# A gated mixture of experts behind an attention stage: table reads moved to the head of each tile, half a weight matrix asked for after the hidden rows' way back, four fill products less

## What is computed

```python
for b in range(B):                       # 4
    prev_e = -1
    for s in range(S):                   # 576
        fresh_e = int(np.argmax(logits[b, s]))
        if s == 0 or local_gate[b, s] < 0.5:
            e = fresh_e
        else:
            e = prev_e if prev_e >= 0 else fresh_e
        prev_e = e
        ...
        h = np.maximum(x[b, s] @ w1[e], 0.0)      # 512 -> 1024
        out[b, s] = p[e] * (h @ w2[e])            # 1024 -> 512
```

## Time and profile before

| | |
|---|---|
| median of 3 runs | 449.35 us (448.23 to 450.46) |
| profiled execution, its own time | 446.81 us |
| its span | 445.1 us |
| mean granted clock of TensorE | 0.99 |
| TensorE (PE) busy | 423.7 us, 95% of the span |
| VectorE (DVE) busy | 304.0 us, 68% |
| ScalarE (ACT) busy | 228.8 us, 51% |
| GpSimd (POOL) busy | 306.3 us, 69% |

### The profile page before, as it was taken

One profiled execution on the slowest core, in us unless ns is written; L12 is line 12 of the kernel. 1 busy time (PEld: TensorE's weight loads), 2 busy tenths in 40 slices (PEclk: granted clock), 3 DMA queues, 4 the chain that ended last, 5 costly groups with the idle time before them and its releaser, 6 DMA issues.

```text
span 445.1 us, 13699 instructions
## 1 busy us (share of the span) xinstructions
PE 423.7 (95%) x3938; PEld 338.3 (76%) x3939; DVE 304.0 (68%) x502; ACT 228.8 (51%) x399; POOL 306.3 (69%) x324
## 2 busy tenths in 40 slices
PE   7999999999989989999999999999988979999992
PEld 3888888888768735788888878888867868888882
DVE  5678887887866687875872783786386877847440
ACT  3778777777777313263542742453273656435210
POOL 6877777877889404788777577687678767776421
PEclk9999999999999998999999999999999999999997
DMA  8989999999695675457779759968959999784430
GB/s 173 195 172 196 176 195 172 188 183 194 108 300 139 143 267 186 128 147 238 250 219 343 224 174 306 294 192 268 319 190 278 332 309 325 230 250 139 155 98 34
DMA packets 105740, 93.78 MB, mean 211 GB/s; under 512 B 49430, under 2 KB 84246, under 8 KB 105688
## 3 DMA queue, kind: packets, MB, share of 16 engines
q1 hardware_dynamic: 99960, 81.91, 69.8%
q0 software_dynamic: 5728, 11.30, 8.4%
HBM read 71.66 MB, written 22.82 MB: 212 GB/s over the span
## 4 chain that ended last, share of the span: by engine, by line
PE 72%; DMA 10%; DVE 8%; issue 3%; ACT 3%; SPq 2%; DVEq 1%; ACTq 1%; POOL 0%; POOLq 0%
PE psum L1689 39%; DMA h_part<-h_rows 5%; PE psum L1413 5%; PE psum L1486 4%; PE psum L1395 4%; DMA h_rows<-tile_bufs 3%; PE psum L1501 3%; PE psum L1449 2%; PE psum L1515 2%; PE psum L1423 2%; PE psum L1579 2%; DVE w_ring L1272 2%; PE psum L1472 2%; PE psum L1462 2%; PE psum L1590 2%
## 5 line engine op out<-in xcount | busy, mean ns | idle before, releaser
L749 POOL DMA_INDIRECT tile_bufs<-x_rows,from_part x96 | 128.4, 1337 | 49.2 <-issue 26.5
L1689 PE MATMUL psum<-w_ring,xg_t 128*128 x552 | 130.4, 392 | 2.9 <-DVE w_ring L1272 2.3
L1689 PE MATMUL psum<-w_ring,h_t 128*128 x552 | 130.2, 392 | 2.8 <-DVE w_ring L1272 2.3
L1689 PEld LDWEIGHTS psum<-w_ring,xg_t 128*128 128x128 f32 x552 | 103.2, 188 | 26.9 <-issue 5.3
L1689 PEld LDWEIGHTS psum<-w_ring,h_t 128*128 128x128 f32 x552 | 103.5, 188 | 26.2 <-issue 3.8
L1272 DVE TENSOR_TENSOR w_ring<-w_ring (+1 forms) x28 | 63.4, 2292 | 28.7 <-ACT w_ring L927 21.9
L970 ACT CAST h_t<-h_raw 128x512 fp32r<-128x512 f32 x46 | 27.3, 621 | 65.9 <-DVE h_raw L1298 65.9
L1298 DVE STREAM_TRANSPOSE h_raw<-h_part 128x512 f32<-128x512 f32 x46 | 29.9, 688 | 41.7 <-DMA h_part<-h_rows 41.7
L755 POOL DMA_INDIRECT out<-tile_bufs,to_row x23 | 29.9, 1301 | 25.5 <-DVE tile_bufs L1313 18.4
L962 ACT ACTIVATE tile_bufs<-psum 128x512 f32<-128x512 f32 x46 | 24.9, 594 | 40.5 <-PE psum L1689 38.3
L927 ACT CAST w_ring<-w_ring (+1 forms) x14 | 26.6, 1910 | 17.8 <-issue 14.7
(11 more groups left out here) (186 smaller groups left out, 620.7 us busy)
## 6 DMA issues: line engine op xcount, KB each, us to landing
w_ring<-moe_w SPq DMA_DIRECT2D x28, 1024.0 KB, 8.9
h_rows<-tile_bufs SPq DMA_DIRECT2D x46, 256.0 KB
h_part<-h_rows SPq DMA_DIRECT2D x92, 128.0 KB
early<-q SPq DMA_DIRECT2D x32, 144.0 KB, 4.1
early<-k SPq DMA_DIRECT2D x32, 144.0 KB, 4.0
early<-v SPq DMA_DIRECT2D x16, 288.0 KB
x_rows<-early SPq DMA_DIRECT2D x48, 96.0 KB, 2.6
early<-v SPq DMA_DIRECT2D x32, 120.0 KB
```

Of the source, the lines that this page charges most:

```text
L749: pool.indirect_dma_start(xg[:, t % 2, s * 128:(s + 1) * 128], None, x_parts[:, :], bass.IndirectOffsetOnAxis(from_part[:, t, s:s + 1], 0) ...
L1689: ins = mm(bank[b][:, :], rows, w_ring[:, bass.ds(at + (off + c * width + n * 512), 512)], start=(c == 0 and k == 0), stop=(c == chunks - ...
```

## The change

Three edits. SP, ScalarE and VectorE read all table entries of a tile at its head, ahead of all its work, instead of one by one ahead of each part that they decide; the reads of the late half of W2, W1 and the early half are kept in registers until used. In SP's `tile` the issue of `rest` stands behind `h_back` and no longer behind `h_store`. `WARM_TILES` is 18 instead of 22. TensorE's program is otherwise the same.

```diff
-    WARM, WARM_FIRST, WARM_CODES, WARM_HELD, WARM_TILES = 8, 4, 10, 4, 22
+    WARM, WARM_FIRST, WARM_CODES, WARM_HELD, WARM_TILES = 8, 4, 10, 4, 18
...
             def tile(t, par, w1=True, w2=True, rest=None):
 
+                if w1:
+                    next_w1 = next_of(t + 1)
+                if w2:
+                    next_w2 = next_of(t - 1)
                 h_store(t, par)
-                if rest:
-                    load_half_w2(1, par, *rest)
...
                 if w1:
 
-                    e, at = next_of(t + 1)
-                    load_next(load_w1, s_w1_in, 1 - par, e, at, 0, 1)
+                    load_next(load_w1, s_w1_in, 1 - par, *next_w1, 0, 1)
                 h_back(t, par)
+                if rest:
+                    load_half_w2(1, par, *rest)
                 if w1:
-                    load_next(load_w1, s_w1_in, 1 - par, e, at, 1, PIECES)
+                    load_next(load_w1, s_w1_in, 1 - par, *next_w1, 1, PIECES)
                 if w2:
 
-                    e, at = next_of(t - 1)
                     wait(sp, s_y, t - 1)
-                    load_half_w2(0, 1 - par, e, at)
-                    return e, at
+                    load_half_w2(0, 1 - par, *next_w2)
+                    return next_w2
...
-            def half_next_w2(t, piece, par, tiles):
+            def next_of(t):
 
-                e = act.value_load(tab_next[0:1, one(t)], min_val=0, max_val=E - 1)
+                return (act.value_load(tab_next[0:1, one(t)], min_val=0, max_val=E - 1),
+                        act.value_load(tab_next_w[0:1, one(t)], min_val=0, max_val=PLACE))
+
+            def half_next_w2(whose, piece, par, tiles):
+
+                e, at = whose
                 with act.If(e != 0):
-                    half_w2_hi(piece, par, tiles, act.value_load(tab_next_w[0:1, one(t)], min_val=0, max_val=PLACE))
+                    half_w2_hi(piece, par, tiles, at)
...
             def tile(t, par, half, x=True, w=True, late=True):
 
+                if late:
+                    late_w2 = next_of(t - 3)
+                if w:
+                    next_w1 = next_of(t)
+                next_w2 = next_of(t - 2)
                 relu(t, par)
                 h_hi(t - 1, 1 - par)
                 if x:
                     x_hi(t + 2, par)
 
                 if late:
-                    half_next_w2(t - 3, 1, 1 - par, half - 1 + par)
+                    half_next_w2(late_w2, 1, 1 - par, half - 1 + par)
                 if w:
-                    split_next_hi(t, half + 1, s_w1_in[par], s_w1_hi, 0, W1C)
-                half_next_w2(t - 2, 0, par, half)
+                    split_next_hi(next_w1, half + 1, s_w1_in[par], s_w1_hi, 0, W1C)
+                half_next_w2(next_w2, 0, par, half)
```

More of the change, by code:

```diff
@@ L928, in half_w2_hi, with split_next_hi @@
                                w_ring[:, bass.ds(at + (WCOLS + W1C + piece * n), n)].bitcast(F32)).then_inc(s_w2_hi, 1)
-            def half_next_w2(t, piece, par, tiles):
-                e = act.value_load(tab_next[0:1, one(t)], min_val=0, max_val=E - 1)
+            def next_of(t):
[3 more added lines that the diff above has]
+                e, at = whose
                 with act.If(e != 0):
-                    half_w2_hi(piece, par, tiles, act.value_load(tab_next_w[0:1, one(t)], min_val=0, max_val=PLACE))
-            def split_next_hi(t, tiles, s_in, s_hi, at, cols):
-                e = act.value_load(tab_next[0:1, one(t)], min_val=0, max_val=E - 1)
+                    half_w2_hi(piece, par, tiles, at)
+            def split_next_hi(whose, tiles, s_in, s_hi, at, cols):
+                e, place = whose
                 with act.If(e != 0):
-                    split_hi(s_in, s_hi, tiles,
-                             act.value_load(tab_next_w[0:1, one(t)], min_val=0, max_val=PLACE) + at, cols)
+                    split_hi(s_in, s_hi, tiles, place + at, cols)
             def first_x_hi():
@@ L988, in _ @@
             x_hi(3, 1)
-            split_next_hi(1, 1, s_w1_in[1], s_w1_hi, 0, W1C)
+            split_next_hi(next_of(1), 1, s_w1_in[1], s_w1_hi, 0, W1C)
             for i in range(PIECES):
@@ L1018, in _ @@
                     h_hi(t - 1, (t - 1) % 2)
-                    half_next_w2(t - 3, 1, (t - 1) % 2, (t - 1) // 2)
+                    half_next_w2(next_of(t - 3), 1, (t - 1) % 2, (t - 1) // 2)
                     for i in range(PIECES):
-                        half_next_w2(t - 2, i, t % 2, t // 2)
+                        half_next_w2(next_of(t - 2), i, t % 2, t // 2)
         @block.vector
@@ L1273, in split_lo, with next_of, split_next_lo @@
                                             ALU.subtract).then_inc(s_lo, 1)
-            def split_next_lo(t, s_hi, s_lo, at, cols, first=0, end=PIECES):
-                e = dve.value_load(tab_next[0:1, one(t)], min_val=0, max_val=E - 1)
+            def next_of(t):
+                return (dve.value_load(tab_next[0:1, one(t)], min_val=0, max_val=E - 1),
+                        dve.value_load(tab_next_w[0:1, one(t)], min_val=0, max_val=PLACE))
+            def split_next_lo(whose, s_hi, s_lo, at, cols, first=0, end=PIECES):
+                e, place = whose
                 with dve.If(e != 0):
-                    split_lo(s_hi, s_lo, e,
-                             dve.value_load(tab_next_w[0:1, one(t)], min_val=0, max_val=PLACE) + at, cols, first, end)
+                    split_lo(s_hi, s_lo, e, place + at, cols, first, end)
             def x_tr(t, par, came):
@@ L1326, in tile @@
                 if late:
-                    split_next_lo(t - 3, s_w2_hi, s_w2, W1C, W2C, 1, PIECES)
+                    split_next_lo(late_w2, s_w2_hi, s_w2, W1C, W2C, 1, PIECES)
                 y_scale(t - 2, par, half)
                 if w:
-                    split_next_lo(t, s_w1_hi, s_w1, 0, W1C)
-                split_next_lo(t - 2, s_w2_hi, s_w2, W1C, W2C, 0, 1)
+                    split_next_lo(next_w1, s_w1_hi, s_w1, 0, W1C)
+                split_next_lo(next_w2, s_w2_hi, s_w2, W1C, W2C, 0, 1)
             x_tr(1, 1, 1)
@@ L1365, in _ @@
             x_lo(3, 1)
-            split_next_lo(1, s_w1_hi, s_w1, 0, W1C)
+            split_next_lo(next_of(1), s_w1_hi, s_w1, 0, W1C)
             split_lo(s_w2_hi, s_w2, 1, PLACE + W1C, W2C)
@@ L1381, in _ @@
                     h_lo(t - 1, (t - 1) % 2)
-                    split_next_lo(t - 3, s_w2_hi, s_w2, W1C, W2C, 1, PIECES)
+                    split_next_lo(next_of(t - 3), s_w2_hi, s_w2, W1C, W2C, 1, PIECES)
                     y_scale(t - 2, t % 2, t // 2 - 1)
-                    split_next_lo(t - 2, s_w2_hi, s_w2, W1C, W2C)
+                    split_next_lo(next_of(t - 2), s_w2_hi, s_w2, W1C, W2C)
                     y_scale(t - 1, (t - 1) % 2, (t - 1) // 2)
```

## The result

Over 20 executions each, the changed kernel has a median of 453.75 us (448.47 to 457.43) and the kernel before 449.05 (447.32 to 458.05). The ratio is 1.0059, 95% interval 1.0031 to 1.0087: slower by 0.6%. The forecast was 443.3, with a range up to 447.4.

The account below looks back on a forecast made before the run. TensorE was busy 95% of the span, so only its idle time at three breaks could be won. -6.3 (breaks) + 0.4 (S(17)) - 0.1 (fills) = -6.0 us from the 449.35 median gave 443.3, range 440.3 to 447.4.

Parts of the forecast that it names:

- I book the reads at nothing by themselves, and 0.8 us more slack at every break.: Reads at tile heads were taken as covered by waits, costing nothing; SP's earlier W1 issue adds 0.8 us slack.
- F(2): First product of slot tile 2; four fills less were to bring it at most 0.24 us, booked as 0.1.
- S(17): Second product of slot tile 17, with 0.3 us of slack before the change; a loss of 0.4 was booked.
- ScalarE's row of 0.89: ScalarE's 0.89 us idle on issue between x cast and late-half weight cast, to vanish with the reads moved.
- The heads of the tiles are not covered: Rival, chance 0.06: six reads ahead of relu and the h_part transpose cost up to 3.3 us each; time 453.
- S(15): Second product of slot tile 15, the third break: 2.45 us lost before, waiting for the second matrix's split.
- F(15): First product of slot tile 15, the second break: 2.51 us lost before, to be covered by 3.2 won.
- SP's order at S(6): First break, second product of slot tile 6: rest behind h_part wins 3.2 us against 0.61 lost; the wait goes.
- Break three goes, or a remnant of up to 1 us stays: At S(15), h_part lands 3.5 us earlier and the rest near 357, so its 2.45 us loss goes or nearly.
- The late half of W2 becomes the bound: Rival, chance 0.17: rest 2 to 3 us later, S(15) keeps 2.45, S(17) waits 1; time 446.8.
- The fills: Four fill products fewer before the first products: worth 0.8 us there, of which 0.1 was booked.
- The sum: Over the whole kernel: -6.3 (breaks and after-effects) + 0.4 (S(17)) - 0.1 (fills) = -6.0 us.

Follow-up runs that it names:

- i1: VectorE's reads at the heads of the tiles and nothing else, against the kernel before: ratio 1.0303.
- i2: VectorE's and ScalarE's reads at the heads; SP, order and fills as in the kernel before: ratio 1.0087 to it.
- e2: The kernel before with only the rest issued behind h_back instead of behind h_store: ratio 0.9904 to the kernel before.
- f3: The order alone again, the same edit as e2, in another group: ratio 0.9931 to the kernel before.
- h3: The changed kernel with ScalarE's reads back where they stood: ratio 1.0188 to the kernel before.
- g2: The new order of SP and 18 fills, all reads where they stood before: ratio 0.9961 to the kernel before.
- h4: g2 again in another group, order and 18 fills with no read moved: ratio 0.9940 to the kernel before.
- g3: The changed kernel with the rest back behind the store, so reads at the heads and 18 fills: ratio 1.0033 to the kernel before.
- g1: The changed kernel with 22 fills instead of 18, so reads at the heads and the new order: ratio 0.9977 to the kernel before.
- f1_after: The changed kernel measured again: median 472.30 us, ratio 1.0060 to the kernel before.
- h1: The changed kernel measured again in another group: median 467.41 us, ratio 1.0014 to the kernel before.

## Why the prediction was wrong, step by step

- **"I book the reads at nothing by themselves, and 0.8 us more slack at every break."** This is the step that failed. A head was to cost up to 3.3 us only where it is not covered, with "up to 1 us of lateness" in tiles without weights. It is uncovered on VectorE in 14 tiles at 2.6 us and on ScalarE in 13 at 2.1, and every kernel of the table above with moved reads takes 3.8 us or more longer from F(2) to the end. The queue does run ahead, but not far enough. This is the chain after, ahead of S(17):

```profile
381.39 0.31 DVEq L1397
...
382.10 0.30 DVEq L1290
...
382.72 0.30 DVEq L1291
...
383.69 0.30 DVEq L1290
...
384.30 0.30 DVEq L1291
...
384.91 0.31 DVEq L1290
...
385.53 0.31 DVEq L1291
```

The three splits before it work until 384.29 (they began at 377.60 and take 6.69). L1397 is the read of the number of tiles in use, which stands once behind the loop in both kernels, at 381.39, 2.9 us under the splits. The six reads of the head (L1290 and L1291 in turn) start at 382.10, 2.2 us under them. A read mostly follows the last one by 0.61 us, and the six take 4.1; the transposition starts at 386.23, 1.9 after the splits' end. My single row of a read under a working engine showed that cover exists, not how much of it. The Trainium skill, "DMA: Bandwidth & Descriptors", section "Latency and other measured facts", has about 600 ns as the floor of a tensor_load. The pace here, 0.61 with the register work, comes out at that, though the load's own row is 0.30 to 0.31. My 0.55 was a little low.

- **What the reads left.** I looked at where the reads go and not at what covered them where they stood. VectorE's were free there, in the wait for ScalarE's cast. I had credited only ScalarE's row of 0.89. i1 against i2 shows both sides: VectorE's move costs 3.0%, ScalarE's gives 2.1% back.
- **The slower rival, "The heads of the tiles are not covered"**, had the right place, a price near the measured one (2 to 3 us at breaks; S(15) lost 3.3 more, S(17) 2.1, F(15) gained 0.5) and a time of 453, which is what came, at a chance of 0.06. That its time fits so well is in part luck: its 10 us were to fall on four places, and fell mostly on S(15), the product behind it and S(17). My evidence against it was again that one row.
- **SP's order at S(6): right.** h_part was transposed at 242.80 (before 245.48), the late half cast at 246.06 (2.9 sooner than in the earlier trace rows; the sum said 3.6), and the wait is gone, though not in e2, f3 and h3 (0.8 to 1.9 late). At F(15) it is right in g2 (0.5 lost) and e2 (0.1), and not in f3 and h4 (4.0 and 4.9 lost), for which I have no cause; in the changed kernel F(15) still loses 2.05.
- **"Break three goes, or a remnant of up to 1 us stays": wrong even for the order alone.** The rest was issued at 351.75 in g2, as worked out (351.8), but landed at 359.3 and not near 357: I gave it a slot of 3.4 to 4 behind h_part, and it took 7.5 us from issue to landing. (No row shows the 1.8 us that I gave h_part at the least; the shortest landing that the list of issues of the trace before gives is 2.0.) S(15) kept its loss (3.0), S(17) lost 1.6 and not 0.4. That is the first rival, "The late half of W2 becomes the bound", in the numbers it gave: break three kept, a wait of 1 at S(17). In the mechanism it is right at S(15) only; at S(17) in g2 it was the store issued behind the rest, which took 6.00 us, where my sum had a slot of 1.5, read from no row. The rival's -2.6 us is also near g2's measured -0.4% (1.8 us), but that is not borne out: by g2's own profile breaks and after-effects took 0.5 us more than before, not 2.6 less. Where its 0.4% comes from is not shown.
- **The two rivals met, in one profile.** Behind h_back the rest hangs on relu and the store. In the profile after, relu's reads made the store of that tile 2.5 us later than before, and the rest 2.3 later than in g2; it also landed 0.8 us more slowly, and S(15) loses 5.74 instead of 3.0. Without the new order (g3) the weights of S(15) are ready 3.9 us sooner after F(15). But g1, with the same reads and order, loses no more at S(15) than g2. That the meeting costs something beyond the two parts is argued from these traces, not shown. How the parts add up stays open too: the reads of all three engines alone gave 0.9971 and 0.9949 on chips with pauses, and with 18 fills on a chip without them 1.0033, while without SP's (i2) they gave 1.0087. SP's own heads or the chips may be the difference; no run had SP's heads alone, and none had all reads alone on a chip without pauses.
- **The fills: right that they are worth nothing** (1.0035, an interval that takes in 1, and the same 19.73 us from the first fill to F(2)). The 18 took 4.07 us, 0.23 each against 0.30 before, the granted clock from 176 to 189 was 1.00, and F(2) started at 188.5.
- **The sum** took each break from the execution profiled before and moved it. No term was for a chain that is free today becoming late, apart from the 0.4 at S(17), and that is where 3.3 (S(15)) + 1.7 (behind it) + 2.1 (S(17)) of the loss came from.

The version that beats both kernels is the order without the reads: 0.9904 and 0.9931 with 22 fills, 0.9961 and 0.9940 with 18. The last two are the firmer ones, as their medians of all executions say the same (0.4 and 0.8% below before).

## What to carry to other kernels

Before moving a small instruction to a "free" place, ask what covers it where it stands: VectorE's reads in the shadow of a wait cost nothing here, and the same reads ahead of the engine's first work of a tile stopped it for 2.6 us on average in 14 tiles. A transfer that is issued behind another step is issued late when that step is late, so an edit that delays relu and an edit that puts a load behind relu's store must be judged together. And time the parts of a change apart: here one of three was worth 0.4 to 1.0% by the ratios, and the reads hid it.

## What the runs showed of the hardware

Long waits of TensorE cost more than their length here. These are the windows of the changed kernel around S(15) (stretch: us, busy time and instructions of PE, PEld, DVE, ACT, POOL, granted clock, DMA share, GB/s):

```profile
360.00:365.00 5.00, 1.60 (x8) 0.98 (x6) 2.09 (x4) 2.44 (x2) 3.43 (x4) 0.94 0.94 310
365.00:370.00 5.00, 2.78 (x7) 2.21 (x8) 2.53 (x2) 1.08 (x2) 4.07 (x3) 0.50 1.03 236
370.00:375.00 5.00, 5.00 (x21) 4.04 (x20) 2.18 (x4) 1.44 (x3) 0.72 (x1) 0.88 1.03 335
```

After 5.62 us of idle TensorE the granted clock is 0.50, the level of 1.2 GHz, and S(15) takes 2.0 us more. In g3, F(15) after an idle time of 3.25 takes 8.30 to the next start, 2.8 more (granted clock 0.59 from 340 to 345). In the kernel before an idle time of 2.33 cost 0.47 more, and one of 2.34 cost 0.25.

The chips differ by more than the edits: the same kernel before has a median of 449 to 451 us in three of the measurements and 466 to 470 in three others. In those TensorE stops within products, as this wait of f1_after shows (us in total, times, longest):

```profile
PE psum L1712 <- issue: 17.9, 19, 5.7
```

In the profile after, from the first measurement, that wait is 0.2 us. In e2, f3, h1 and h4 it is 13.1, 10.7, 11.2 and 5.4. I have no experiment on its cause. The difference makes ratios from different chips comparable only roughly; on the slower ones part of the time in which weights are late may lie under these pauses, which could be why the changed kernel measured only 1.0014 on one of them.
